# A rational gate in a fused attention and two-layer kernel: 512 columns at a time in place of 2 x 256, with other waits

## The reference

```python
h = x @ w_in                                              # layer one
g = np.maximum(h, 0.0) + alpha * np.minimum(h, 0.0)
x = g @ w_out

h = x @ w_in                                              # layer two
h2 = h * h
h3 = h2 * h
P = a[0] + a[1] * h + a[2] * h2 + a[3] * h3
Q = 1.0 + np.abs(b[0]) * np.abs(h) + np.abs(b[1]) * h2
g = P / (Q + 1e-06)
return g @ w_out
```

## Time and profile before

| what | value |
|---|---|
| median of 3 runs | 693.26 us (693.15 to 693.6) |
| profiled execution | 695.82 us, span 694.1 us |
| mean granted TensorE clock | 0.977 of full speed |
| PE busy | 653.2 us (94%), 3072 matmuls |
| DVE busy | 542.3 us (78%), 922 instructions |
| ACT busy | 380.9 us (55%), 948 instructions |
| POOL busy | 308.7 us (44%), 369 instructions |
| DMA | 31.32 MB, 45 GB/s on the mean |

### The profile page before, as it was taken

One profiled execution on the slowest core, in us unless ns is written; L12 is line 12 of the kernel. 1 busy time (PEld: TensorE's weight loads), 2 busy tenths in 40 slices (PEclk: granted clock), 3 DMA queues, 4 the chain that ended last, 5 costly groups with the idle time before them and its releaser, 6 DMA issues.

```text
span 694.1 us, 10389 instructions
## 1 busy us (share of the span) xinstructions
PE 653.2 (94%) x3072; PEld 509.7 (73%) x3072; DVE 542.3 (78%) x922; ACT 380.9 (55%) x948; POOL 308.7 (44%) x369
## 2 busy tenths in 40 slices
PE   4776999999999999999999998999999999999994
PEld 3554777777777777778888886777777777778873
DVE  8997666666566666745555479999999999999995
ACT  4765233233223333322111187888898888899992
POOL 4649300000000000000444478777777777798882
PEclk9986899999999999999999999999999999999999
DMA  7664011110001102001222210000010000100001
GB/s 205 195 191 135 18 46 28 31 50 26 28 5 49 26 26 53 9 0 61 92 91 92 92 61 0 1 1 1 1 60 0 0 0 0 60 2 1 1 1 64
DMA packets 38937, 31.32 MB, mean 45 GB/s; under 512 B 9008, under 2 KB 33264, under 8 KB 38896
## 3 DMA queue, kind: packets, MB, share of 16 engines
q1 hardware_dynamic: 38896, 30.83, 14.8%
HBM read 27.67 MB, written 3.15 MB: 44 GB/s over the span
## 4 chain that ended last, share of the span: by engine, by line
PE 49%; POOL 25%; DVE 13%; issue 7%; ACT 4%; POOLq 1%; DMA 0%; SPq 0%; DVEq 0%; ACTq 0%
PE ps_h L541 20%; PE ps_y L564 19%; POOL numer L1170 8%; POOL denom L1168 8%; POOL numer L1172 8%; PE ps_s L487 4%; PE ps_o L513 3%; DVE denom L967 3%; PE ps_o L502 2%; DVE prob L913 1%; DVE rowmax L893 1%; DVE xy_raw L913 1%; DVE g_lo L977 1%; DVE numer L970 1%; ACT p_low L704 1%
## 5 line engine op out<-in xcount | busy, mean ns | idle before, releaser
L967 DVE RECIPROCAL denom<-denom 128x256 f32<-128x256 f32 x96 | 167.2, 1742 | 3.8 <-POOL denom L1168 3.8
L1160 POOL TENSOR_TENSOR win_lo<-stage,win_hi 128x1024 fp32r<-128x1024 f32 x8 | 19.2, 2403 | 276.4 <-DVE win_hi L936 276.4
L541 PE MATMUL ps_h<-xy_hi,win_hi 128*128 (+1 forms) x288 | 120.0, 417 | 0.7 <-DVE xy_lo L925 0.7
L541 PE MATMUL ps_h<-xy_lo,win_hi 128*128 (+1 forms) x288 | 113.7, 395 | 0.0
L541 PE MATMUL ps_h<-xy_hi,win_lo 128*128 (+1 forms) x288 | 113.4, 394 | 0.0
L683 ACT ACTIVATE g_hi<-g 128x512 fp32r<-128x512 f32 x48 | 30.3, 631 | 136.6 <-PE ps_y L564 129.2
L1168 POOL TENSOR_TENSOR denom<-denom,q_abs 128x256 f32<-128x256 f32 x96 | 78.1, 813 | 45.4 <-ACT denom L708 41.6
L566 PE MATMUL ps_y<-wout_hi,g_hi 128*128 128x512 f32 x192 | 79.2, 413 | 10.4 <-DVE g_lo L977 8.4
L953 DVE TENSOR_TENSOR g_lo<-g,g_hi 128x512 fp32r<-128x512 f32 x48 | 33.2, 693 | 66.0 <-ACT g_hi L683 66.0
L564 PE MATMUL ps_y<-g_hi,wout_hi 128*128 128x512 f32 x192 | 80.8, 421 | 0.0
L1170 POOL TENSOR_TENSOR numer<-numer,h_sq 128x256 f32<-128x256 f32 x96 | 78.0, 813 | 0.0
(11 more groups left out here) (132 smaller groups left out, 1334.8 us busy)
## 6 DMA issues: line engine op xcount, KB each, us to landing
stage<-in_w_in SPq DMA_DIRECT2D x8, 512.0 KB, 3.4
stage<-in_w_out SPq DMA_DIRECT2D x8, 512.0 KB, 3.4
qT<-in_q SPq DMA_DIRECT2D x48, 64.0 KB, 2.5
kT<-in_k SPq DMA_DIRECT2D x24, 128.0 KB, 2.4
vv<-in_v SPq DMA_DIRECT2D x24, 128.0 KB, 2.2
out<-xy_raw SPq DMA_DIRECT2D x12, 256.0 KB, 2.2
xy_raw<-in_w_in SPq DMA_DIRECT2D x4, 512.0 KB, 5.1
xy_raw<-in_w_out SPq DMA_DIRECT2D x4, 512.0 KB, 4.4
```

The costliest lines, as they stand in the source:

```text
L541: mm = pe.matmul(ps_h_at(layer, m), w[:, kc, cut], x[:, blk, kc, :], start=(kc == 0 and n == 0), stop=(kc == KC - 1 and n == 2))
L967: dve.reciprocal(denom[:, r, :], denom[:, r, :]).then_inc(inverse_ready, 1)
```

## The change

Layer two's gate works on whole tiles of 512 columns. The buffers keep their total size (`h_sq`, `p_low`, `q_abs` one of 512; `numer` and `denom` two of 512). ACT's order becomes square, magnitude, `denom`, `numer`, `p_low`, and each has a wait of its own: the square for POOL's multiplication of the step before, the magnitude for POOL's addition to `denom` of the step before, `denom` for DVE's product two steps back, `numer` for `g_lo` two steps back, `p_low` for POOL's last addition of the step before. DVE does `split2` of the step before, then `inverse2` and `ratio2` of its own. TensorE waits once a tile for `g`, and for `h_read` per tile. At the handover from layer one DVE's reciprocal and product of step 1 stand whole behind `end1`; before, the first half stood ahead of it.

```diff
-            h_sq = sb("h_sq", [P, 2, HALF], F32, second)
-            p_low = sb("p_low", [P, 2, HALF], F32, second)
-            q_abs = sb("q_abs", [P, 2, HALF], F32, second)
-            numer = sb("numer", [P, 4, HALF], F32, second)
-            denom = sb("denom", [P, 4, HALF], F32, second)
+            h_sq = sb("h_sq", [P, TOK], F32, second)
+            p_low = sb("p_low", [P, TOK], F32, second)
+            q_abs = sb("q_abs", [P, TOK], F32, second)
+            numer = sb("numer", [P, 2, TOK], F32, second)
+            denom = sb("denom", [P, 2, TOK], F32, second)
...
# TensorE
-                        pe.wait_ge(h_read, c2 * 2 - 6)
+                        pe.wait_ge(h_read, c2 - 3)
...
-                if layer == 1:
-                    pe.wait_ge(g2_ready, 2 * MC * blk + (2 * m + half + 1))
+                if half == 0 and layer == 1:
+                    pe.wait_ge(g2_ready, MC * blk + (m + 1))
...
# ACT
-            def gate2(blk, m, half):
...
-                if not (isinstance(u, int) and u < 2):
-                    act.wait_ge(numer_ready, u - 1)
-                    act.wait_ge(denom_ready, u - 1)
-                if not (isinstance(u, int) and u < 4):
-                    act.wait_ge(g2_ready, u - 3)
...
+            def gate2(blk, m):
+                u, r = MC * blk + m, m % 2
...
+                ph = ps_h_at(1, m)
+                if not (isinstance(u, int) and u == 0):
+                    act.wait_ge(numer_high, u)
+                act.wait_ge(h_done, MC * blk + (m + MC * BLOCKS + 1))
+                act.activation(h_sq[:, :], ph, ACT.Square).then_inc(square_ready, 1)
+                if not (isinstance(u, int) and u == 0):
+                    act.wait_ge(denom_ready, u)
+                act.activation(q_abs[:, :], ph, ACT.Abs, scale=ab_sb[:, 6:7]).then_inc(abs_ready, 1)
                 if not (isinstance(u, int) and u < 2):
+                    act.wait_ge(ratio_ready, u - 1)
+                act.wait_ge(square_ready, u + 1)
+                act.activation(denom[:, r, :], h_sq[:, :], ACT.Identity, scale=ab_sb[:, 7:8],
+                               bias=ab_sb[:, 8:9]).then_inc(denom_square, 1)
+                if not (isinstance(u, int) and u < 2):
+                    act.wait_ge(g2_ready, u - 1)
                 act.activation(numer[:, r, :], ph, ACT.Identity, scale=ab_sb[:, 3:4],
+                               bias=ab_sb[:, 2:3]).then_inc(line_ready, 1)
+                if not (isinstance(u, int) and u == 0):
+                    act.wait_ge(numer_ready, u)
+                act.activation(p_low[:, :], ph, ACT.Identity, scale=ab_sb[:, 1:2],
+                               bias=ab_sb[:, 0:1]).then_inc(h_read, 1)
+
+            def split2(blk, m):
+                act.wait_ge(ratio_ready, MC * blk + (m + 1))
+                act.wait_ge(y_done, MC * blk + (m + MC * BLOCKS - 1))
+                act.activation(g_hi[:, m % 2, :], numer[:, m % 2, :], ACT.Copy).then_inc(g2_hi_ready, 1)
...
-                        for half in range(2):
-                            gate2(blk + arg // MC, arg % MC, half)
-                            split2(*before(blk, arg), half)
+                        gate2(blk + arg // MC, arg % MC)
+                        split2(*before(blk, arg))
...
# DVE
+            def inverse2(blk, m):
+                r = m % 2
+                dve.wait_ge(denom_ready, MC * blk + (m + 1))
                 dve.reciprocal(denom[:, r, :], denom[:, r, :]).then_inc(inverse_ready, 1)
+
+            def ratio2(blk, m):
+                r = m % 2
+                dve.wait_ge(inverse_ready, MC * blk + (m + 1))
+                dve.wait_ge(numer_ready, MC * blk + (m + 1))
                 dve.tensor_tensor(numer[:, r, :], numer[:, r, :], denom[:, r, :], ALU.mult).then_inc(ratio_ready, 1)
 
+            def split2(blk, m):
+                r = m % 2
+                dve.wait_ge(ratio_ready, MC * blk + (m + 1))
+                dve.wait_ge(g2_hi_ready, MC * blk + (m + 1))
+                dve.tensor_tensor(g_lo[:, r, :], numer[:, r, :], g_hi[:, r, :].bitcast(F32),
+                                  ALU.subtract).then_inc(g2_ready, 1)
+
+            def gate2(blk, m):
+
+                split2(blk + (m - 1) // MC, (m - 1) % MC)
+                inverse2(blk, m)
+                ratio2(blk, m)
...
+                elif what == "g" and arg == MC:
+                    inverse2(0, 0)
+                    ratio2(0, 0)
                 elif what == "g" and arg == MC + 1:
 
-                    gate2(0, 1, 0)
-                    split2(0, 0, 1)
+                    split2(0, 0)
...
                     end1(BLOCKS - 1)
-                    gate2(0, 1, 1, low_part=False)
+                    inverse2(0, 1)
+                    ratio2(0, 1)
...
# POOL
+                u, r = MC * blk + m, m % 2
+                top, under = numer[:, r, :], denom[:, r, :]
+                pool.wait_ge(abs_ready, u + 1)
+                pool.wait_ge(denom_square, u + 1)
+                pool.tensor_tensor(under, under, q_abs[:, :], ALU.add).then_inc(denom_ready, 1)
+                pool.wait_ge(line_ready, u + 1)
+                pool.tensor_tensor(top, top, h_sq[:, :], ALU.mult).then_inc(numer_high, 1)
+                pool.wait_ge(numer_high, u + 1)
+                pool.wait_ge(h_read, u + 1)
+                pool.tensor_tensor(top, top, p_low[:, :], ALU.add).then_inc(numer_ready, 1)
```

More of the change, by code:

```diff
@@ L217, in build_program @@
         y_read = sem("y_read")
-        parts_ready = sem("parts_ready")
+        square_ready = sem("square_ready")
+        abs_ready = sem("abs_ready")
+        line_ready = sem("line_ready")
         numer_high = sem("numer_high")
@@ L683, in split1 @@
                 act.activation(g_hi[:, m % 2, :], g1[:, :], ACT.Copy).then_inc(g_hi_ready, 1)
-            def gate2(blk, m, half):
-                u = 2 * MC * blk + 2 * m + half
-                r = 2 * (m % 2) + half
+            def gate2(blk, m):
+                u, r = MC * blk + m, m % 2
                 if isinstance(u, int) and u == 0:
@@ L702, in gate2 @@
-                act.activation(numer[:, r, :], ph, ACT.Identity, scale=ab_sb[:, 3:4],
[L703 to L717, removed]
+                ph = ps_h_at(1, m)
+                if not (isinstance(u, int) and u == 0):
+                    act.wait_ge(numer_high, u)
@@ L755, in _ @@
                 if what == "g" and arg >= MC:
-                    for half in range(2):
-                        gate2(0, arg - MC, half)
-                        if arg > MC:
-                            split2(0, arg - MC - 1, half)
+                    gate2(0, arg - MC)
+                    if arg > MC:
+                        split2(0, arg - MC - 1)
                 elif what == "split" and arg < MC:
@@ L768, in _ @@
                             end2(blk)
-                        for half in range(2):
-                            gate2(blk + arg // MC, arg % MC, half)
-                            split2(*before(blk, arg), half)
+                        gate2(blk + arg // MC, arg % MC)
+                        split2(*before(blk, arg))
             for what, arg in block_events(1, False, None):
                 if what == "g":
-                    for half in range(2):
-                        gate2(BLOCKS - 1, arg, half)
-                        split2(BLOCKS - 1, arg - 1, half)
+                    gate2(BLOCKS - 1, arg)
+                    split2(BLOCKS - 1, arg - 1)
                     if arg == MC - 1:
-                        for half in range(2):
-                            split2(BLOCKS - 1, arg, half)
+                        split2(BLOCKS - 1, arg)
             for j in range(0, KC, 2):
@@ L1040, in _ @@
                     if what == "g":
-                        for half in range(2):
-                            gate2(blk + arg // MC, arg % MC, half)
+                        gate2(blk + arg // MC, arg % MC)
             for what, arg in block_events(1, False, None):
                 if what == "g":
-                    for half in range(2):
-                        gate2(BLOCKS - 1, arg, half)
-            for half in range(2):
-                split2(BLOCKS - 1, MC - 1, half)
+                    gate2(BLOCKS - 1, arg)
+            split2(BLOCKS - 1, MC - 1)
             for j in range(1, KC, 2):
@@ L1162, in gate2 @@
             def gate2(blk, m):
-                for half in range(2):
-                    u, r = 2 * MC * blk + (2 * m + half), 2 * (m % 2) + half
-                    top, under = numer[:, r, :], denom[:, r, :]
-                    pool.wait_ge(denom_square, u + 1)
-                    pool.tensor_tensor(under, under, q_abs[:, half, :], ALU.add).then_inc(denom_ready, 1)
-                    pool.wait_ge(parts_ready, u * 3 + 3)
-                    pool.tensor_tensor(top, top, h_sq[:, half, :], ALU.mult).then_inc(numer_high, 1)
-                    pool.wait_ge(numer_high, u + 1)
```

(3 more changed lines are left out.)

19 lines of the change are left out of this document (removed).

## The result

The changed kernel takes 696.8 us in the median of 18 runs (695.82 to 699.51), the kernel before 693.2 beside it (690.57 to 696.76): a ratio of 1.0053, 95% interval 1.0038 to 1.0068. It is slower by 3.6 us; 695.2 was forecast, +2.0.

The account below looks back on a forecast made before the run. DVE's loop was taken to bound the looped blocks, TensorE the last. Handover, steps of 5.68 and borders put the last product +0.9 late, the tail added +1.1: +2.0, 695.2 us; case range 691 to 699, reaching toward 684 and 703.

Parts of the forecast that it names:

- the case named likeliest: Whole kernel: DVE and POOL exclude each other, steps of 5.68, +2.0 us to 695.2; chance 0.66, own range 691 to 699.
- What bounds the kernel: Layer two before: DVE's loop sets the looped blocks at 5.83 a step, 0.9 from POOL; TensorE's 5.44 sets the last.
- Prices at 512 columns: Layer two's gate instructions: reciprocal 3.26, DVE product 0.72, g_lo record 0.69, POOL record 1.29, copy to g_hi 0.63.
- the reciprocal's bounds: DVE's 512-column reciprocal: 3.26 expected, 3.32 as bound above; 3.33 would make the step 5.74, +2.6.
- The loop: Layer two's steps: 1.70 + 3.26 + 0.72 = 5.68, gaining 0.15 in looped blocks, losing 0.24 in the last.
- Start: Handover from layer one: product 3 ends at 433.6 against 432.89 before, 0.7 late.
- Borders: Two block borders: ACT's output copies delay POOL, so products end at 6.27 and 6.23; 1.14 each, 2.3 for both.
- Tail: Last product to the last twelve matmuls: 1.51 in place of 0.39, as g_lo is no longer in halves; +1.1.
- New waits at no cost: ACT's new waits in layer two, such as the denominator's on the product two steps back, cost nothing.
- the faster one: Layer two: POOL's numerator addition not ahead of g_lo, steps about 5.44, 681 us; chance 0.16.
- The lost race: Layer two: POOL's addition starts before DVE's product, mean step 6.29, +0.61 for 44 steps, 722 us; chance 0.13.
- the prediction's rule for two inputs: DVE and POOL: a DVE operation with two SBUF inputs and a POOL operation shut each other out whole.

Follow-up runs that it names:

- experiment 9: The kernel before, with its half reciprocals written into the hidden tile's PSUM bank, so each product has one SBUF input: 675.75 us, ratio 0.9744.
- Experiment 8: The changed kernel with ACT's four output copies of a block behind the next tile's gate instead of ahead of it: 694.24 us, ratio 1.0013.
- Experiment 1: The changed kernel with the reciprocal written into the hidden tile's PSUM bank, so the product has one SBUF input: 687.65 us, ratio 0.9922.
- experiment 3: The changed kernel with POOL's addition of q_abs done on 384 of the 512 columns: 709.64 us, ratio 1.0239.
- experiment 2: The changed kernel with the product written to PSUM and read there by ACT's copy and g_lo, the reciprocal staying in SBUF: 692.92 us, ratio 0.9994.
- experiment 4: The changed kernel with POOL's addition of q_abs done on 448 of the 512 columns: 694.77 us, ratio 1.003.
- experiment 5: The changed kernel with ACT's old order (square, numerator line, p_low, magnitude, denominator) and its waits: 734.25 us, ratio 1.0592.
- experiment 6: The changed kernel with g_lo of the step before moved behind the next reciprocal, all in SBUF: 686.67 us, ratio 0.9904.
- experiment 7: The changed kernel with reciprocal and product in PSUM, g_lo behind the next reciprocal, and ACT's numerator wait on g_lo removed: 682.27 us, ratio 0.9846.

## Why the prediction was right

The direction, the mechanism and the case named likeliest were right; the size was 2.0 for 3.6.

- *What bounds the kernel.* Right of the looped blocks: experiment 9 takes one of the product's two SBUF inputs away and the 0.9 with it. Of the last block it was too simple: I gave it to TensorE alone, but DVE went through it without a pause too, at 5.46, with the port in each product.
- *Prices at 512 columns.* Right to 0.02: reciprocal 3.34 a record (3.26 behind its forerunner), products 0.69, POOL 1.29, copy 0.63. Neither end of the reciprocal's bounds was needed. (In the earlier trace rows DVE's subtraction ends 1.09 after POOL's addition, where I wrote 1.11; nothing rests on it.)
- *The loop.* Forecast 5.68, measured 5.69; the product's start forecast at 4.99, measured 5.00; g_lo 0.55 behind POOL; POOL's addition 1.66 for "near 1.7". TensorE's pause, forecast as 0.24 a step, shows as 0.34 to 0.38 idle in the rows of its weight loads; what makes it longer isn't shown. The hundredth in the step is 0.5 us in the end.
- *Start.* Forecast 433.6 for product 3, measured 433.70. But products 4 and 5 took 5.73 and 5.74, where I had 5.60 and 5.68: +0.2.
- *Borders.* The mis-sized term. I gave 1.14 each. The first takes 6.44 + 6.38 - 2 x 5.69 = 1.44, the second 1.36: 2.80 for 2.3. POOL's denominator addition starts 4.60 after the product there, not 4.43, and the product ends 0.55 after it, as forecast (the first border):

```profile
512.39 1.29 POOL L1164 TENSOR_TENSOR denom<-denom,q_abs 128x512 f32<-128x512 f32 x1 [3.45 <-ACT denom L705]
...
512.78 1.45 DVE L963 TENSOR_TENSOR numer<-numer,denom 128x512 f32<-128x512 f32 x1
```

Experiment 8 takes the border steps down to 5.70 to 5.74. The three steps behind the first border are another 0.15 over; experiment 8 leaves them as they are, and their cause is open.
- *Tail.* Forecast 1.51, measured 687.13 to 688.64, 1.51; the row of the chain, of before:

```profile
688.64 3.07 PE ps_y L568 x12
```

- *New waits at no cost.* No row of the changed kernel shows ACT idle ahead of its denominator, and its product two steps back ends at 543.52 for a denominator at 545.14. No run leaves that wait out.

Of 3.6 us, then, the sum held 2.0; borders (0.5), the hundredth (0.5), the first steps (0.2), the three behind the first border (0.15) and the handover (0.1) are some 1.4 of the other 1.6. That is all that the two traces differ by up to the last twelve matmuls (3.4 for 2.0); another 0.3 lies behind these and wasn't followed.

The rivals: the faster one (g_lo not behind POOL, 681) did not come. Experiment 1 comes nearest to the state it described, at 5.52 a step and 687.65 us. So that rival was priced too low by some 6 us: it had 5.45 a step and 0.5 for both borders, where experiment 1 takes 1.1 at each. The lost race did not come either, by 0.19 us (548.52 against 548.71; I had given 0.14), and experiment 3 made it come by taking work away. There it cost 0.41 a step (the mean of 5.44 and 6.75, less 5.69), not the 0.61 that the rival was priced at: the step after a lost race ran at 5.44, where I had 5.60.

The rule of the Trainium skill on instruction size (VectorE: DVE Perf Modes, TRN2 errata) is true here of the work, some 21 us less for DVE, and says nothing of the time: against the saved starts stand the 0.77 that DVE now waits for a copy each step, and POOL instructions of 1.29 in place of 0.74 to stand behind. The rule of the Trainium skill on the shared port (SBUF — State Buffer, Who interferes with whom) gave the right outcome: experiments 1 to 3 agree that the first to start holds the other up for its whole instruction. The runs show the exclusion; that it is a port is the Trainium skill's account.

## What to carry to other kernels

Look for records of one operation that come in two lengths. Where DVE's long ones end a fixed time after a POOL instruction (0.28 or 0.55 us here), suspect that the two shut each other out. Here an input moved to PSUM, in a bank whose tile is already read, freed both, and that was worth 2.6% where reshaping the gate cost 0.5%. When two engines take turns at a resource, shorter or longer instructions decide who comes first, so bigger tiles, or less work, can cost: follow one period by hand to the instruction that starts next, and give the margin of each race. And before an instruction is made larger, ask who waits for its first half.

## What the runs showed of the hardware that was not expected

- 128 columns less of a POOL addition, 0.27 us, made the kernel 12.8 us slower (experiment 3): start times 0.08 apart decide it, as did 0.05 the other way (experiment 4).
- PSUM costs DVE nothing here, as output or as input: reciprocals of 3.35 to PSUM against 3.34, products and g_lo of 0.69 either way.
- A conversion of one input takes part in the exclusion too, which the prediction's rule for two inputs leaves out, though its sum for the handover counts on it (such a conversion pushed to 426.6; measured 426.71). In the earlier trace rows DVE's 1024-column conversion and POOL's addition both start at 424.72, and POOL's ends 0.60 after DVE's; in the changed kernel that conversion lasts 1.79 in place of 0.68 and ends 0.56 after a POOL addition. The reciprocal, also of one input, stops nobody.
- One profiled execution and the next differ before layer two: product 0 ended between 405.5 and 409.4 us in kernels whose first 400 us have the same code. Below half a per cent, single spans mislead. The stretch from product 0 to 47 is a better guide: its differences agree with those of the medians within 1 us in experiments 1 to 4, 8 and 9, and within 3 us in experiments 5 to 7.
